# Attention and two FFN layers in one kernel: every attention matmul in 64-row tiles, values in two parts, a new order of work

## The reference

```python
q_rot, k_rot = (rotate(q), rotate(k))
scores = scale * np.matmul(q_rot, k_rot.transpose(0, 1, 3, 2))
scores = scores - np.max(scores, axis=-1, keepdims=True)
attn = np.exp(scores)
attn = attn / (np.sum(attn, axis=-1, keepdims=True) + 1e-09)
out = np.matmul(attn, v)
x = out.transpose(0, 2, 1, 3).reshape(B * S, H * D)
h = x @ w_in;  g = h - np.tanh(h);             x = g @ w_out      # first layer
h = x @ w_in2; g = h * (1 / (1 + np.exp(-h))); x = g @ w_out2     # second layer
```

## Time and profile before

| | us |
|---|---|
| median of three runs | 1110.88 (1110.35 to 1112.07) |
| the profiled execution, its own time | 1111.94 |
| its span, first to last instruction | 1110.1 |
| TensorE busy in it | 1075.9 (97%) |
| VectorE, ScalarE, GpSimd busy | 443.0, 419.5, 282.6 |
| attention, up to the first FFN matmul | 301.35 |

### The profile page before, as it was taken

How to read it: one execution, slowest core, us unless ns; L and a number is a source line. 1 busy time by engine, 2 the same in 40 slices (tenths; PEclk the granted TensorE clock), 3 DMA queues, 4 the chain that set the end, 5 groups by cost and what they waited for, 6 DMA issues and landing times.

```text
span 1110.1 us, 16519 instructions
## 1 busy us (share of the span) xinstructions
PE 1075.9 (97%) x6608; PEld 987.7 (89%) x6608; DVE 443.0 (40%) x712; ACT 419.5 (38%) x775; POOL 282.6 (25%) x121
## 2 busy tenths in 40 slices
PE   2899999999999999999999999999999999999998
PEld 1778888888899999999999999899999999899997
DVE  5566666666253323223232333623223232322322
ACT  1567686676722323223232322323223232232322
POOL 5776978873551000000000015700000000000000
PEclk9999999999999999999999999999999999999999
DMA  5344446532152000000000004200000000000000
GB/s 182 133 154 146 133 127 217 162 102 71 29 168 76 1 1 0 0 0 0 0 0 0 0 0 151 76 1 29 0 0 28 0 28 0 0 28 0 29 0 28
DMA packets 36331, 58.35 MB, mean 53 GB/s; under 512 B 15680, under 2 KB 17984, under 8 KB 34368
## 3 DMA queue, kind: packets, MB, share of 16 engines
q1 hardware_dynamic: 36288, 57.78, 16.0%
HBM read 48.37 MB, written 4.79 MB: 48 GB/s over the span
## 4 chain that ended last, share of the span: by engine, by line
PE 89%; POOL 5%; DVE 2%; DMA 1%; ACT 1%; issue 1%; SPq 0%; ACTq 0%; POOLq 0%; DVEq 0%
PE ps L597 35%; PE ps L616 18%; PE ps L611 17%; PE ps L535 6%; PE ps L501 4%; PE ps L466 2%; PE ps L530 2%; PE ps L527 1%; PE ps L503 1%; PE ps L493 1%; POOL wout_l L399 1%; POOL hl L379 1%; POOL win_l L399 1%; DVE hm L777 1%; POOL raw L374 1%
## 5 line engine op out<-in xcount | busy, mean ns | idle before, releaser
L597 PE MATMUL ps<-xs_h,win_l 128*128 128x384 f32 x768 | 258.6, 337 | 1.4 <-DVE xs_l L834 1.4
L597 PE MATMUL ps<-xs_h,win_h 128*128 128x384 f32 x768 | 257.6, 335 | 0.0
L597 PE MATMUL ps<-xs_l,win_h 128*128 128x384 f32 x768 | 257.1, 335 | 0.0
L742 ACT ACTIVATE g_h<-ps 128x384 fp32r<-128x384 f32 x192 | 94.5, 492 | 306.3 <-PE ps L616 135.1
L736 ACT ACTIVATE act<-ps 128x384 f32<-128x384 f32 x192 | 94.5, 492 | 247.6 <-PE ps L597 247.4
L597 PEld LDWEIGHTS ps<-xs_h,win_l 128*128 128x128 f32 x768 | 144.2, 188 | 7.5 <-issue 3.9
L597 PEld LDWEIGHTS ps<-xs_l,win_h 128*128 128x128 f32 x768 | 144.2, 188 | 3.5
L597 PEld LDWEIGHTS ps<-xs_h,win_h 128*128 128x128 f32 x768 | 144.1, 188 | 0.0
L777 DVE TENSOR_REDUCE hm<-ps 128x2 f32<-128x576 f32 x144 | 108.5, 756 | 79.8 <-PE ps L466 77.9
L399 POOL TENSOR_TENSOR win_l<-w_stage,win_h 128x2048 fp32r<-128x2048 f32 x8 | 39.6, 4953 | 350.2 <-DVE win_h L830 344.5
L611 PE MATMUL ps<-g_h,wout_h 128*128 128x384 f32 x384 | 128.3, 334 | 0.0
(11 more groups left out here) (75 smaller groups left out, 1523.5 us busy)
## 6 DMA issues: line engine op xcount, KB each, us to landing
raw<-qk SPq DMA_DIRECT2D x15, 1152.0 KB, 6.5
w_stage<-w_in SPq DMA_DIRECT2D x8, 1024.0 KB, 5.1
w_stage<-w_out SPq DMA_DIRECT2D x8, 1024.0 KB, 5.4
R<-inverse_sums SPq DMA_DIRECT2D x32, 144.0 KB, 3.1
v<-vfull SPq DMA_DIRECT2D x16, 256.0 KB, 2.9
out<-ostage SPq DMA_DIRECT2D x5, 768.0 KB, 3.6
vr<-vin SPq DMA_DIRECT2D x16, 192.0 KB, 3.2
ev<-ev SPq DMA_DIRECT2D x16, 144.0 KB, 2.3
```

Of the source, the lines that this page charges most:

```text
L597: last = mm(o, w[g][:, kk, c:c + 128], x[:, kk, :], start=(n == 0), stop=(n == 11))
L742: nc.scalar.activation(g_h[f % 2][:, :], ps[:, 4 + f % 4, 0:TN], ACT.Copy, scale=(1.0, 0.5)[L]).then_inc(s_gh, 1)
```

## The change

- **64-row tiles throughout.** The values of a unit of 128 keys are computed in two parts (`phase` 0 and 1). In the first, the lower 64 keys go with head 0 into bank 6 while the upper 64 go with head 1 into bank 7; in the second, the banks are crossed. The rest scores, the rest row scores and the transposes are cut in the same way. Between a first and a second part TensorE waits on a semaphore of its own (`s_pa`, `s_sa`, `s_xa`, and `s_pv` before the next first part), and other work, mostly scores, is put there. Only units 5 to 8 of the last pair stay whole (`weigh_at_once`).
- **A new order on TensorE**, written out step by step, with 17 named places for row scores, each a single one from pair 4 on (`X_STEADY`); the turn is behind scores 7 (8 for pairs 0 and 1).
- **VectorE**: one maximum or two between the low parts; `invert` behind the low part of unit 7, ahead of the maxima of the places S8 and A6.
- **ScalarE**: the first half of the queries is moved out between the two exps of unit 7; the second half of the pair before is moved out behind unit 1; high parts of q, k, v and of the weights stand elsewhere, the weights' in single quarters for pairs 3 to 10.
- **GpSimd and SP**: low parts of weights in quarters; `rope_scale` ahead of `v_low`; the inverse is spread in the iteration after; the maxima go out ahead of the rest blocks' copies.
- **Start**: six loads (cosines, q, sines, swapped q, k, swapped k) with a semaphore each; ScalarE takes the high part of q while VectorE rotates k. Row score (1, 0) no longer stands ahead of scores (0, 0).

The core of the diff:

```diff
-        WEIGHED = [(0, None), (2, 0), (1, None), (3, None), (4, None), (2, 1), (5, None), (6, None), (7, None), (8, None)]
+        WEIGHED = [(2, 0), (0, None), (1, None), (3, None), (4, None), (2, 1), (5, None), (6, None), (7, None), (8, None)]
+        X_STEADY = {"B6": 1, "A8": 1, "S5": 1, "B1": 1, "A3": 1, "S7": 1, "S8": 1, "A6": 1}
+        X_REST = [("S7", "S8")] + [("RA", "RB")] * (PAIRS - 2)
+        X_TURN = [8, 8] + [7] * (PAIRS - 3)
...
-            sp.dma_start(stab[:, 0, :], sinq).then_inc(s_tab, 16)
-            sp.dma_start(ctab[:, 0, :], cosq).then_inc(s_tab, 16)
-            for i in range(2):
-                sp.dma_start(raw[0][:, i:4:2, :], qk[0, :, i:4:2, :]).then_inc(s_ld0[i], 16)
+            sp.dma_start(ctab[:, 0, :], cosq).then_inc(s_tab[0], 16)
+            sp.dma_start(raw[0][:, 0, :], qk[0, :, 0, :]).then_inc(s_ld0[0], 16)
+            sp.dma_start(stab[:, 0, :], sinq).then_inc(s_tab[1], 16)
+            sp.dma_start(raw[0][:, 2, :], qk[0, :, 2, :]).then_inc(s_ld0[2], 16)
+            sp.dma_start(raw[0][:, 1, :], qk[0, :, 1, :]).then_inc(s_ld0[1], 16)
+            sp.dma_start(raw[0][:, 3, :], qk[0, :, 3, :]).then_inc(s_ld0[3], 16)
...
+            def weigh(n, u, phase):
...
+                else:
+                    p, t = ring(g), SPLIT.index(i)
+                    for m, (w, x) in enumerate(((vh, pl), (vl, ph), (vh, ph))):
+                        for r, a in enumerate(heads):
+                            h = r ^ phase
+                            last = mm(ps[:, OB + h, 0:HALF], w[n % 2][a, t, h, :], x[p][a, h, :],
+                                      start=(first and m == 0), stop=False)
...
+                scores(n, 0).then_inc(s_st, 1)
+                x_place(n, "S0")
+                if n:
+                    pe.wait_ge(s_pa, 4 * n - 1)
+                    other_keys(n - 1, (5, 6))
+                x_place(n, "B6")
+                scores(n, 1).then_inc(s_st, 1)
+                x_place(n, "S1")
+                if n:
+                    pe.wait_ge(s_pv, 10 * n - 2)
+                    weigh(n - 1, 7, 0)
+                    weigh(n - 1, 8, 0).then_inc(s_pa, 1)
+                x_place(n, "A8")
+                scores(n, 2, 0).then_inc(s_sa, 1)
+                x_place(n, "RA")
+                if n:
+                    pe.wait_ge(s_pa, 4 * n)
+                    other_keys(n - 1, (7, 8))
+                scores(n, 2, 1).then_inc(s_st, 1)
+                x_place(n, "RB")
+                scores(n, 3).then_inc(s_st, 1)
+                weigh(n, 0, 0)
+                scores(n, 4).then_inc(s_st, 1)
+                x_place(n, "S4")
+                weigh_rest(n, 0)
+                weigh(n, 1, 0).then_inc(s_pa, 1)
+                x_place(n, "R0")
+                scores(n, 5).then_inc(s_st, 1)
+                x_place(n, "S5")
+                pe.wait_ge(s_pa, 4 * n + 1)
+                other_keys(n, (0, 1))
+                x_place(n, "B1")
+                scores(n, 6).then_inc(s_st, 1)
...
+                x_place(n, "S8")
...
+                weigh_rest(n, 1)
+                if more:
+                    weigh(n, 5, 0)
+                    weigh(n, 6, 0).then_inc(s_pa, 1)
+                x_place(n, "A6")
...
                     nc.scalar.activation(ph[ring(g)][:, :, :], s, ACT.Exp, scale=SCALE).then_inc(s_ex, 1)
+                    if between is not None:
+                        move_out(n, between)
                     nc.scalar.activation(s, s, ACT.Exp, scale=SCALE).then_inc(s_ex, 1)
...
+                x_place(n, "S7", "B4")
+                low(9 * n + 7)
+                invert(n - 1)
+                x_place(n, "S8", "A6")
```

More of the change, by code:

```diff
@@ L470, in max_transpose, with scores @@
             def max_transpose(n, bank):
                 pe.wait_ge(s_nm, n + 1)
-                return nc.tensor.transpose(ps[0:UNITS, bank, 288:416], negmax[n % 2][:, :], idf[:, :])
-            def scores(n, u):
+                for h, a in enumerate(heads):
+                    last = nc.tensor.transpose(ps[0:UNITS, bank + h, 288:352], negmax[n % 2][a, :], idf[a, a])
+                return last
+            def scores(n, u, phase=0):
                 g = 9 * n + u
@@ L507, in scores_done, with ready @@
                 last.then_inc(s_st, 1)
-            def weigh(n, u, half=None):
+            def ready(n, u):
                 g = 9 * n + u
-                qh, i = S_UNITS[u]
                 if is_full(g):
@@ L515, in weigh @@
                     pe.wait_ge(s_lo, splits_to(g + 1))
-                first, final = (u, half) in ((0, None), (2, 1)), u in (4, 8)
                 if u == 0:
@@ new lines, in weigh_at_once @@
+            def weigh_at_once(n, u):
+                g = 9 * n + u
+                i = S_UNITS[u][1]
+                ready(n, u)
+                if is_full(g):
+                    for h in range(2):
+                        last = mm(ps[:, OB + h, 0:HALF], v1[n % 2][:, 0, h, :], P[:, h, :], start=False, stop=u in (4, 8))
+                else:
+                    p, t = ring(g), SPLIT.index(i)
+                    for m, (w, x) in enumerate(((vh, pl), (vl, ph), (vh, ph))):
+                        for h in range(2):
+                            last = mm(ps[:, OB + h, 0:HALF], w[n % 2][:, t, h, :], x[p][:, h, :],
+                                      start=(u == 0 and m == 0), stop=False)
+                last.then_inc(s_pv, 1)
@@ L537, in weigh, with other_keys, x_place @@
-                last.then_inc(s_pv, 1)
-            def weigh_last(n):
-                if n >= 0:
-                    weigh(n, 7)
-                    weigh(n, 8)
+                for h, a in enumerate(heads):
+                    last = mm(ps[:, OB + h, 0:HALF], v1[n % 2][a, 1, h, :], PR[a, half, :], start=(half == 1), stop=False)
+                last.then_inc(s_pv, 1)
+            def other_keys(n, units):
+                for u in units:
+                    weigh(n, u, 1)
+            def x_place(n, name):
+                for x in x_places[n, name]:
+                    row_scores(x)
@@ new lines, in _ @@
+                x_place(n, "A4")
+                last = scores(n, 7)
+                if more and X_TURN[n] == 7:
+                    last = turn(n, 7)
+                last.then_inc(s_st, 1)
+                x_place(n, "S7")
+                pe.wait_ge(s_pa, 4 * n + 2)
+                other_keys(n, (3, 4))
+                x_place(n, "B4")
+                last = scores(n, 8)
+                if not (more and X_TURN[n] == 8):
+                    last.then_inc(s_st, 1)
+                x_place(n, "S8")
@@ L583, in ffn_tile @@
+                if more and X_TURN[n] == 8:
+                    turn(n, 8).then_inc(s_st, 1)
+                weigh_rest(n, 1)
[3 more added lines that the diff above has]
+                x_place(n, "A6")
+            for u in (5, 6, 7, 8):
+                weigh_at_once(PAIRS - 1, u)
             def ffn_tile(L, T):
@@ L666, in exps @@
                 sc.wait_ge(s_st, g + 1)
-                if turn is not None:
-                    copy_rows(turn, bank + 1)
+                if n + 1 < PAIRS and X_TURN[n] == u:
+                    copy_rows(n + 1, bank)
                 s = ps[:, bank:bank + 2, 0:HALF]
```

336 lines of the change are left out of this document (185 added, 151 removed), and 3 rows, old and new, of the table X_RAMP.

## The result

| | before | after |
|---|---|---|
| median of four runs, us | 1111.47 (1110.35 to 1112.55) | **1128.60** (1128.22 to 1129.39) |
| the profiled execution, its own time; its span | 1111.94; 1110.1 | 1128.48; 1126.6 |
| first scores of pair 0 | 26.21 | 22.31 |
| a middle pair (4 to 13) | 16.53 | 17.84 |
| first FFN matmul | 301.35 | 317.86 |

The ratio is 1.0155, with a 95% interval of 1.0137 to 1.0173: 1.5% slower, where 1124 us was forecast. All of it is there when FFN starts: 16.5 us in the profiled executions, which are 16.5 us apart as wholes.

A forecast was written before the change was run, and what follows sets the result against it. TensorE, with 89% of the last-ending chain, was taken to bound the kernel. Start -3.8, ramp +3.1, middle pairs +12.9 and last pairs +1.0 gave +13.2 on 1111.94, 1.06 above the median: 1124 us, range 1107 to 1132.

The forecast's parts named there:

- part 3: Ramp and end: pairs 0 to 3 take 79.7 us against 76.65, +3.1; pairs 14 and 15 add +1.0.
- Part 1, tiles: All eight tile-height switches of a pair go, 24.5 us over 16 pairs; slots stay at 14.24 us a pair.
- Part 2, waits: New engine orders add waits: a middle pair takes 17.82 us against 16.53, ten pairs +12.9 us.
- The walk: Step-by-step timing of one middle pair through TensorE, VectorE and ScalarE hand-overs in series, giving 17.82 us.
- Step 7: End of a middle pair: last row waits 1.1 us for S8's maximum, behind low part 7 and inverse on VectorE.
- steps 4 and 5: Mid-pair: scores 5 wait for scores 3's banks until 8.65 us; the row after next waits for its maximum, ending at 10.57.
- not its load but its order binds: VectorE in middle pairs: by its share it would carry an 11 us pair, so its list order sets the time.
- the clock might fall behind waits: Rival: half clock after each new 1.1 us gap costs a pair 1 to 2 us, 1133 to 1155 us; chance 0.05.
- Part 4, start: Before pair 0: reordered loads and row scores bring first scores from 26.21 to 22.4, -3.8 us (bounds -1.5 and -4.5).
- Other queues: GpSimd, weight quarters on ScalarE and SP's copies are covered and cost nothing, at most +-1 us.
- The drains decide, faster: Rival between scores and values: only today's 0.7 us waits remain, pair 14.9, 1084 us; chance 0.17 for anything below 1108.6.
- Half of the waits: Rival at the pair's end: VectorE's wait shorter by inverse and one maximum (1.1 us), pair 16.7, 1110 to 1116; chance 0.13.

The follow-up runs named there:

- the first experiment: Changed kernel with VectorE's maximum of the place S8 row moved ahead of the low part of unit 7 and the inverse: 1115.86 us, ratio 1.0045.
- all repairs: Changed kernel with S8's maximum earlier, S5's row ahead of scores 5 (pairs 1 to 3 too), and pair 1's rest rows earlier in pair 0: 1110.82 us, ratio 0.9993.
- the first two experiments: Changed kernel with S8's maximum ahead of low part 7: 1115.86 us; that kernel with S5's row scores also ahead of scores 5: 1111.26 us, ratio 1.0001.

## Why the prediction was right

**The sum.** By its own terms, all from the first scores and the first FFN matmul:

| | predicted | measured |
|---|---|---|
| start | -3.8 | -3.9 |
| pairs 0 to 3 | +3.1 | +5.8 |
| ten middle pairs | +12.9 | +13.1 |
| pairs 14 and 15 | +1.0 | +1.5 |
| sum | +13.2 | +16.5 |

With 1111.94 for the profiled run before it gives 1128.4, and the profiled run after took 1128.48. The forecast's step that was mis-sized is the ramp (part 3).

**Part 1, tiles.** Right: slots of 0.131 and 0.242, all eight switches gone, no price for crossed banks. The saving was there, 24.5 us of switches at the price read from the trace before. That they cost what was said the whole transposes show: two of them take 0.35 us, where 0.20 and 0.14 were read. The Trainium skill ("TensorEngine Tiling (Array Packing)", Key Properties) has the drain at a change of mode, with which the trace agrees: 0.20 us at a change of tile height before, none where the height stays.

**Part 2, waits.** The walk gave 17.82 us a pair, and the trace shows 17.84. Its waits, each the time from one group's end to the next's beyond the slots (the predicted ones worked out from the walk's times):

| ahead of | predicted | measured |
|---|---|---|
| rest scores | 0.30 | 0.44 |
| rest row | 0.30 | 0.25 |
| scores 5 | 0.57 | 0.54 |
| B1 row | 0.34 | 0.33 |
| A3 row | 0.21 | 0.29 |
| scores 7 | 0.26 | 0.17 |
| S7 row | 0.08 | 0.08 |
| rest values (move-out) | 0.36 | 0.50 |
| last row | 1.15 | 0.90 |
| sum | 3.57 | 3.50 |

The single terms are off by up to 0.25, in both directions, so that the sum agrees to 0.07 is in part luck. In part it is not: a wait that ends later shortens the next one on the same chain. Ahead of the last row 0.25 less was waited, and 0.14 of that is the later coming of the rest values ahead of it. Step 7 as the largest wait is shown by the maximum moved ahead, 0.91 us a pair; steps 4 and 5 by the row moved ahead of scores 5, 0.46 a pair; that VectorE's durations are in the path, by the shorter maxima. The prediction set "not its load but its order binds" against the warning of the Trainium skill ("TensorEngine Tiling (Array Packing)", PSUM Bottleneck) that the emptying of PSUM may become the bound. The first experiment bears that out: with the same work in another order 12.7 us came back, 9.0 of them in the middle pairs.

**Part 3, ramp: the term that was mis-sized.** Pairs 0 to 3 were put at +3.1 and measured +5.8. Pair 0 was put at 22.8 and took 24.64, pair 1 at 19.4 and took 19.85, pair 2 at 19.6 and took 19.97; pair 3 was right. The idle wait ahead of the turn was foreseen (2.6, measured 2.40). What it did to the clock was not in the sum: 0.3 us in pair 0, and the 0.4 by which pair 1 is too long (19.44 where the clock stays up). In the rivals stood that the clock might fall behind waits, and was priced only for the 1.1 us wait in the middle pairs, where it didn't fall; the longer wait in the ramp, which the same text named, was not asked that question. The larger part of pair 0's 1.84 us seems to be the slots of 0.24 us up to about 34 us: in two executions where they end 2 to 3 us sooner, scores 5 come 1.0 and 1.1 us sooner. The prediction gives 22.8 without its steps, so what it had assumed there can't be told. The half microsecond left of pair 0, and pair 2, stay open.

**Part 4, start.** -3.9 against -3.8, with some luck. The recorded terms don't add up to the recorded figure: 24.7 less 1.8 and less 0.3 is 22.6, not 22.4, so they give -3.6. And 0.55 of the measured 3.9 is scatter of the first row scores, as said above. The loads brought these 1.8 us forward (12.25 for 14.08), which is the 1.8 of the walk; from there to the first scores the copies save 0.55 and the order 1.0.

**Other queues.** GpSimd and SP cost nothing that shows: the ten middle pairs lie between 17.82 and 17.85. With the early move-out one pair waits about 1 us for the inverse's DMA and GpSimd's product behind it.

**The rivals.** "The drains decide, faster" fell, and how far it was from true is measured: even with the waits of steps 4, 5 and 7 repaired a pair stays at 16.47. It would have had to be 14.9. "Half of the waits" is what the first experiment made: 16.93 and 1115.86, where that rival had 16.7 and 1110 to 1116.

## What to carry to other kernels

Removing a drain or a switch from the engine that bounds the kernel is worth only what the other engines' hand-overs let through: walk once around the period with start-to-start times of every engine in the path, and look at each in-order list for an operation that waits for one engine while finished work of another stands behind it. When a repair of one wait changes nothing, look where the wait reappears before repairing the next; here three further exchanges of order left the pair at 16.54 to 16.93 us, where it had been 16.47. Before a gain is put down to an edit, compare the traces at a place ahead of it. The lowest median of this study has the kernel before with the new start alone, 1109.62 us, 0.12% faster (0.03 to 0.21). That is below the 0.2% that I said could be told from no change, and its interval overlaps that of all repairs (-0.02 to 0.17% faster).

## What the hardware showed that I had not expected

- **Half clock behind one wait, full clock behind others nearly as long.** Behind 2.40 us of idleness ahead of the turn the granted clock was 0.64 and then 0.50 over 4 us, with slots of 0.24 us. The kernel with whole transposes has the same 2.40 and the same fall:

```profile
44.69 0.30 PE L515 MATMUL ps<-idf,negmax 128*9 128x128 f32 x1 [2.40 <-DVE negmax L916]
...
46.00:48.00 2.00, 2.00 (x20) 1.96 (x18) 0.00 (x0) 0.24 (x1) 1.69 (x2) 0.50 0.06 14
```

  With 2.11 us at the same place, in the kernel with shorter maxima, the clock stayed at 1.00:

```profile
41.68 0.22 PE L516 MATMUL ps<-idf,negmax 64*9 64x64 f32 x2 [2.11 <-DVE negmax L919]
...
42.00:44.00 2.00, 1.37 (x18) 1.13 (x16) 0.00 (x0) 1.16 (x3) 0.76 (x1) 1.00 0.01 2
```

  Behind 1.06 us there, in the first two experiments, it stayed up too. What the engine did over the microseconds before the wait differs between these kernels, so this is no threshold.
- **Slots of 0.24 us under a granted clock of 1.00.** Early in an execution TensorE runs slots of 0.24 us while the column of the granted clock shows 1.00. Six score matmuls then last 0.92 us instead of 0.56, in the kernel before at 26.21 and in the changed one still at 32.52:

```profile
32.52 0.92 PE L551 MATMUL ps<-hl 64*128 64x288 f32 x6
```

```profile
32.00:34.00 2.00, 2.00 (x20) 2.00 (x18) 0.03 (x1) 1.46 (x3) 1.92 (x1) 1.00 0.31 111
```

  So here the column does not tell what an early slot costs. Nor does it cancel between kernels. The slots fell to 0.13 us at about 34 us in the changed kernel and with whole transposes, and between 31 and 33.6 us in the executions of the others that share its code up to that place (in the kernel with the rest rows earlier the same six, at 32.43, last 0.56). From the first scores to scores 5 it is 13.13 us in the changed kernel, and 12.04, 12.69 and 12.09 with the maximum first, the row ahead of scores 5 and the rest rows earlier. Each of them is one execution, so whether the kernel or chance sets this is not shown; it puts some 1 us of uncertainty on every comparison of pair 0.
